# Slot 0 read without the plan, half of the plan and the zero blocks in the first layer, spare products on TensorE, and the first turns of the last stage in three banks

## The chip, the cores and the metric

The kernel runs on one core of a Trainium2 chip. The metric is the device time of one execution in microseconds (us). Besides the timed runs there is one profiled execution, whose trace gives all rows below. The engines are PE (TensorE, matrix products), DVE (VectorE), ACT (ScalarE), POOL (GpSimd) and SP (SyncE, which here only issues DMAs).

## The reference

A linear attention with decays, then two mixtures of experts. B, H, S, D = 4, 8, 768, 48, so N = 3072 tokens of 384 numbers; E = 8 experts, hidden width F = 1024.

```python
for t in range(S):                                  # attention
    cur = einsum('bhd,bhe->bhde', u[None] * kt, vt)
    y[:, :, t] = einsum('bhd,bhde->bhe', rt, state + cur)
    state = wt[:, :, :, None] * state + einsum('bhd,bhe->bhde', kt, vt)
...
expert_idx = argmax(logits, axis=1)                 # first layer: best expert of each token
for e in range(E):
    h = maximum(x[expert_idx == e] @ w1[e], 0.0)
    out[expert_idx == e] = gate_w[..., None] * (h @ w2[e])
...
order = argsort(-(x @ w_gate).flatten())            # second layer: pairs by falling logit,
for idx in order:                                   # each expert takes at most N // E tokens
    tok, e = idx // E, idx % E
    if assigned[tok] >= 0 or counts[e] >= cap: continue
    assigned[tok] = e; counts[e] += 1
for e in range(E):
    h = maximum(x[assigned == e] @ w1[e], 0.0)
    out[assigned == e] = h @ w2[e]
```

## The kernel before, in words

The program has three blocks, one behind the other. At the end of a block each engine drains and all five meet; only then does the next block begin. Each engine's program is written out by hand, in order, and engines wait for each other by semaphores. Nothing is planned by a scheduler.

**Attention (lines 153 to 815).** It runs over 24 tiles t of 128 tokens. SP loads decays, k and r, and v. DVE makes two scans of the decays (`scan_after`, `scan_before`), the scaled k (`decay_k`) and the masked scores. POOL makes the scaled r (`decay_r`, line 375). PE makes the scores (`score`, line 687), the outputs (`values`), the state and all turns. POOL begins with a list of constants (lines 330 to 367); only behind the last of them, at line 389, does its loop with `decay_r` begin. Every three tiles DVE chooses the best expert of each token (`choose`) and gives it its place among its expert's rows (`place`). POOL then scatters the rows by an indirect DMA into `sorted_rows` (line 384), which has a region of 3200 rows for each expert. `judge` (line 528) and the product at line 814 find out whether the decays are too wide for this method; if they are, `judged` (line 265) lets all engines run a general form instead. With these inputs it does not.

Behind the last tile DVE runs `plan_slots` (lines 101 to 142): 22 small chained instructions. A slot is a block of 128 rows of one expert, and there are up to 31. The plan gives each slot's expert and first row, each expert's last slot, and in `pad_row` the row behind each expert's last. `pad_regions` (line 145) waits for `pad_row` and stores a block of 128 zero rows behind each expert's rows: SP issues those of experts 0 to 3, ACT those of 4 to 7. SP waits until all eight have landed (line 319), POOL until the last scatters have landed (line 396).

**First layer (lines 1042 to 1337).** It runs over the slots i. SP first raises 26 semaphores (`signals`, line 1110). ACT loads the rows of slot i (`load_x`), whose first row it reads from `slot_row`. PE turns them (line 1275), DVE copies the turn out (line 1230), PE makes the 24 products of the hidden layer (line 1312, in two halves of 12, each product two records), ACT applies relu (line 1171), and PE makes the 8 products of the output (line 1328). DVE's program begins with two fills, `logits` and `tokens`.

**Second layer (lines 1348 to 1860).** It finds the assignment in 8 phases p, one expert each. In a phase DVE offers 31 thresholds at a time (`offer`), PE counts who reaches them (`count`, line 1722), DVE narrows (`narrow`), PE spreads the digit (`digit`, line 1728); four rounds make one threshold. Then PE ranks the members (`rank`), DVE builds `row_is` in two halves (line 1632), PE makes the token table from them (`tables`, line 1744), and POOL gathers the expert's rows from `y_rows` (line 1485). PE turns the three tiles i of 128 rows (`x_transposes`, line 1752), ACT copies them out (`x_evac`, line 1511), and PE makes the expert's two layers (`first`, line 1765, and `second`, line 1781), each product 384 wide. The search of phase p + 1 is written between the products of phase p. For phase 0 there is nothing to put it between. All turns go to the one bank `p_x`, so a turn waits until ACT has copied the last one out.

Of the kernel before, what the change touches and what calls it, by code (L numbers as in the profile page):

```python
# [80 lines left out]
def shared(nc, sb, ps, sem, io, keep):  # L81

    for name, shape, kind in (("ident", [P, P], F32), ("mask", [P, P], F32), ("tri", [P, P], BF16),
# [6 lines left out]
                              ("enT", [P, KD, E], F32), ("bad", [P, 1], I32), ("zeros", [P, ROW], F32),  # L90
# [10 lines left out]
def plan_slots(dve, keep, s_p):  # L101

    base, region, iota8, ones, steps, iota_s = (keep[n] for n in ("base", "region", "iota8", "ones", "steps", "iota_s"))
    slot_expert, slot_row, last_slot, pad_row = (keep[n] for n in ("slot_expert", "slot_row", "last_slot", "pad_row"))
    count, over, slots_of, end_of, start_of = (keep[n] for n in ("count", "over", "slots_of", "end_of", "start_of"))
    past, which, pick, tmp = (keep[n] for n in ("past", "which", "pick", "pick_tmp"))
    start_at, end_at, row_f = (keep[n] for n in ("start_at", "end_at", "row_f"))
    n = [0]

    def chain(ins):  # L110
        n[0] += 1
        ins.then_inc(s_p, 1)
        dve.wait_ge(s_p, n[0])

    by_slot = lambda a: a[:, :].unsqueeze(1).broadcast_to([P, SLOTS, E])
    by_expert = lambda a: a[:, :].unsqueeze(2).broadcast_to([P, SLOTS, E])
    chain(dve.tensor_tensor(count[:, :], base[:, :], region[:, :], ALU.subtract))
    chain(dve.tensor_copy(pad_row[:, :], base[:, :]))
# [4 lines left out]
    chain(dve.tensor_tensor(start_of[:, :], end_of[:, :], slots_of[:, :], ALU.subtract))  # L123
    chain(dve.tensor_tensor(past[:, :, :], by_expert(iota_s), by_slot(end_of), ALU.is_ge))
# [3 lines left out]
    chain(dve.tensor_tensor(pick[:, :, :], by_expert(which), by_slot(iota8), ALU.is_equal))  # L128
# [4 lines left out]

# [6 lines left out]

    chain(dve.tensor_copy(slot_row[:, SLOTS:SLOTS + 1], pad_row[:, E - 1:E]))
    chain(dve.tensor_copy(last_slot[:, :], end_of[:, :]))


def pad_regions(eng, experts, io, keep, s_p, s_pads):

    eng.wait_ge(s_p, 2)
# [5 lines left out]
def attention(nc, general, sb, ps, sem, io, keep):  # L153
# [3 lines left out]
    iota8, region, bad = (keep[n] for n in ("iota8", "region", "bad"))  # L157
# [27 lines left out]
    rows = sb("rows", [P, RB * G, ROW], F32)  # L185
# [8 lines left out]
    pos = sb("pos", [P, RB, G], U32)  # L194
# [15 lines left out]
    s_scale = sem("s_scale")  # L210
# [6 lines left out]
    s_votes = sem("s_votes")  # L217
    s_plan = sem("s_plan")
    s_pads = sem("s_pads")
    s_u = sem("s_u")  # L220
# [54 lines left out]
    with nc.Block() as block:  # L275
# [48 lines left out]
        def _(pool):  # L324
# [40 lines left out]
            for a in range(KD):  # L365
                const(pool.tensor_copy(keep["fold"][32 * a:32 * a + 32, :], ident[32 * a:32 * a + 32, 32 * a:32 * a + E]))
# [1900 lines left out]
```

## Time and profile before

| | us |
|---|---|
| median of 3 timed runs | 880.9 (879.58, 880.90, 883.29) |
| the profiled execution | 879.44 |
| its span, from the first to the last instruction | 877.7 |
| PE busy in the span | 805.9 (92%) |
| DVE busy | 432.7 (49%) |
| ACT busy | 319.2 (36%) |
| POOL busy | 122.4 (14%) |

The span starts at the first instruction; all times in rows count from there. The attention block lasts until about 195 us, the first layer until about 527, the second to the end. Busy times of PE are modelled from pipelined instructions, so a busy PE need not be at its peak.

### The profile page before, as it was taken

Reading aid. Unit: us, or ns where it says so; the run is one execution under the profiler, and the core shown is the slowest. Engines: PE = TensorE matmul, PEld = TensorE weight load, DVE = VectorE, ACT = ScalarE, POOL = GpSimd, SP = SyncE. Lnnn points to the kernel's source line nnn. Section 1 sums busy time; section 2 is a strip of 40 time slices with the busy share of each in tenths; the row PEclk is TensorE's granted clock in tenths of the full one; section 3 lists DMA queues with packets and bytes.
Section 4 is the critical chain, followed back from the end, with each engine's and each line's share of the span. In section 5 each row is a group of like instructions: output and inputs, shape, how many; then the busy total and the mean of one; then the engine's idle time right before and its main releaser. Section 6 shows DMA issues by size and latency. Waiting matters only on the chain. (4 is left out here: it accounts for less than half of the span.)

```text
span 877.7 us, 17862 instructions
## 1 busy us (share of the span) xinstructions
PE 805.9 (92%) x6212; PEld 584.4 (67%) x6213; DVE 432.7 (49%) x1259; ACT 319.2 (36%) x808; POOL 122.4 (14%) x146
## 2 busy tenths in 40 slices
PE   5999999929999999999999982399999999999996
PEld 4888888717877788877788862255565555655653
DVE  7799999742333333333333337664726364452000
ACT  3887788713344443344443340011111112122120
POOL 4123433320000000000000000102021010202201
PEclk9999999968999999999999995599999999999998
DMA  9446555735666555566564520513415051436100
GB/s 303 148 150 203 186 176 183 262 137 178 200 220 236 181 178 189 207 215 238 181 215 150 175 99 2 170 67 124 153 56 177 23 180 53 155 133 215 40 19 29
DMA packets 61918, 136.20 MB, mean 155 GB/s; under 512 B 4696, under 2 KB 36320, under 8 KB 61856
## 3 DMA queue, kind: packets, MB, share of 16 engines
q1 hardware_dynamic: 45536, 98.46, 32.6%
q0 software_dynamic: 6912, 23.75, 7.9%
q10 hardware_dynamic: 9408, 13.18, 4.7%
q8 instruction: 37, 0.61, 0.3%
q14 instruction: 25, 0.20, 0.1%
HBM read 117.48 MB, written 17.89 MB: 154 GB/s over the span
## 5 line engine op out<-in xcount | busy, mean ns | idle before, releaser
L1312 PEld LDWEIGHTS p_h<-x_t,w1s 128*128 128x128 f32 x1296 | 152.3, 193 | 8.0 <-issue 1.1
L1328 PE MATMUL p_o<-w2s,hid_t 128*128 x432 | 156.8, 497 | 0.0
L1312 PE MATMUL p_h<-x_t,w1s 128*128 128x128 f32 x1296 | 154.7, 276 | 0.8 <-DVE x_t L1230 0.8
L1765 PE MATMUL p_gh<-g_t,w1s 128*128 128x384 f32 x384 | 138.1, 506 | 0.7 <-ACT g_t L1511 0.7
L1781 PE MATMUL p_go<-w2s,g_hid 128*128 128x384 f32 x384 | 135.6, 496 | 0.0
L1328 PEld LDWEIGHTS p_o<-w2s,hid_t 128*128 128x128 f32 x432 | 75.8, 190 | 41.2 <-issue 5.2
L1171 ACT ACTIVATE hid_t<-p_h 128x512 f32<-128x512 f32 x54 | 32.2, 597 | 189.2 <-PE p_h L1312 189.2
L1765 PEld LDWEIGHTS p_gh<-g_t,w1s 128*128 128x128 f32 x384 | 71.1, 194 | 43.8 <-issue 5.3
L1781 PEld LDWEIGHTS p_go<-w2s,g_hid 128*128 128x128 f32 x384 | 70.5, 192 | 41.1 <-issue 1.4
L1525 ACT ACTIVATE g_hid<-p_gh 128x384 f32<-128x384 f32 x64 | 31.4, 490 | 122.8 <-PE p_gh L1765 122.8
L1485 POOL DMA_INDIRECT g_in<-y_rows,table x24 | 24.0, 1002 | 254.6 <-DVE table L1640 249.7
L687 PE MATMUL p_g<-r_dec,k_dec 64*128 64x128 f32 x384 | 43.8, 297 | 10.2 <-POOL r_dec L375 9.4
L1518 ACT ACTIVATE o_row<-p_go 128x384 f32<-128x384 f32 x24 | 11.8, 490 | 104.1 <-PE p_go L1781 104.1
L687 PEld LDWEIGHTS p_g<-r_dec,k_dec 64*128 64x128 f32 x384 | 39.0, 199 | 14.1 <-issue 12.6
L425 ACT ACTIVATE diag_v<-v_pad,diag 128x48 f32<-128x48 f32 x192 | 48.0, 327 | 0.0
L1578 DVE TENSOR_TENSOR filled<-p_search,room 31x8 f32<-31x8 f32 x28 | 4.3, 154 | 81.9 <-PE p_search L1722 74.8
L1137 POOL DMA_DIRECT2D w2s<-in_w x12 | 9.1, 757 | 250.2 <-PE p_o L1328 215.9
L375 POOL TENSOR_TENSOR r_dec<-kr_t,decays 128x512 f32<-128x512 f32 x24 | 28.5, 1187 | 104.4 <-issue 60.1
L1722 PEld LDWEIGHTS p_search<-takers,reach 128*31 128x31 bf16 x868 | 23.9, 96 | 25.3 <-DVE reach L1571 13.1
L1495 POOL DMA_INDIRECT out<-o_row,table x24 | 23.5, 978 | 121.6 <-ACT o_row L1518 121.3
L1238 DVE COPY lt<-p_route 96x128 f32<-96x128 f32 x27 | 7.8, 288 | 65.3 <-PE p_route L1290 65.3
L1230 DVE COPY x_t<-p_turn 128x384 f32<-128x384 f32 x28 | 15.6, 558 | 49.1 <-PE p_turn L1275 49.1
(258 smaller groups left out, 1108.3 us busy)
## 6 DMA issues: line engine op xcount, KB each, us to landing
w1s<-in_w SPq DMA_DIRECT2D x28, 1536.0 KB, 6.3
kr_t<-in_kr_t SPq DMA_DIRECT2D x24, 512.0 KB, 4.1
w1s<-in_w1b SPq DMA_DIRECT2D x8, 1536.0 KB, 6.4
w2s<-in_w2b SPq DMA_DIRECT2D x8, 1536.0 KB, 10.6
w2s<-in_w POOLq DMA_DIRECT2D x12, 768.0 KB, 6.7
w_pad<-in_w_t SPq DMA_DIRECT2D x24, 256.0 KB
v_pad<-in_v_pad SPq DMA_DIRECT2D x24, 256.0 KB, 4.3
x_in<-sorted_rows ACTq DMA_DIRECT2D x28, 198.0 KB, 2.5
```

Of the source, the lines that this page charges most:

```text
L375: pool.tensor_tensor(r_dec[:, t % 3, :, :], kr_t[:, q, 1, :, :], before[:, t % 2, :, 0:P], ALU.mult).then_inc(s_rdec, 1)
L425: ins = act.activation(diag_v[:, t % 2, h, :], v_pad[:, q, h, 0:D], ACT.Copy, scale=diag[:, t % 2, h:h + 1])
L687: ins = pe.matmul(p_g[g][:, a, :], k_dec[half, t % 2, a, :], r_dec[half, t % 3, a, :], start=True, stop=True)
L1171: act.activation(hid_t[:, half * g:half * (g + 1), :], p_h[g][:, :, :], ACT.Relu).then_inc(s_relu, 1)
L1312: ins = pe.matmul(p_h[g][:, m, :], w1s[:, q, a, f:f + P], x_t[:, q, a, :], start=(a == 0), stop=(a == KD - 1))
L1328: ins = pe.matmul(p_o[:, :], hid_t[:, m, :], w2s[:, bass.ds(half, 1), m, :].rearrange("p o n -> p (o n)"), start=(m == 0), stop=(m == KF - 1))
L1485: pool.indirect_dma_start(out=x_in[:, i, :], out_offset=None, in_=io["y_rows"][:, :], in_offset=place(0, p, i)).then_inc(s_in[i], 16)
L1495: pool.indirect_dma_start(out=io["out"][:, :], out_offset=place(1, p, i), in_=o_row[:, p % 2, i, :], in_offset=None).then_inc(s_out[p % 2] ...
L1525: act.activation(hid[:, m, :], p_h[(KF * p + m) % 3][:, :], ACT.Relu).then_inc(s_relu, 1)
L1722: ins = pe.matmul(p_c[0:CAND, :], reach[:, i, :], takers[:, i, :], start=(i == 0), stop=(i == SLOTS - 1))
L1765: ins = pe.matmul(p_h[n % 3][:, :], w1s[:, p % 2, a, m * P:(m + 1) * P], x_t[:, a, :], start=(a == 0), stop=(a == KD - 1))
L1781: ins = pe.matmul(p_o[n % 2][:, :], hid[:, m, i * P:(i + 1) * P], w2s[:, p % 2, m, :], start=(m == 0), stop=(m == KF - 1))
```

## The change

- POOL makes `tri`, `cand_0` and `fold` behind its first `decay_r` instead of before it (`later_constants`), and fills `logits` and `tokens` there, which DVE no longer does in the first layer.
- `keep_busy` issues spare f32 products of 128x128x128 whose results nobody reads: 20 at the start of attention, 20 behind the vote, 14 at the start of the first layer, 10, 5 and 15 around the first tables of the second layer.
- The plan is made in three parts: `plan_ends` (pad_row, one step), `plan_slots` (9 steps) in attention, and `plan_rows` (12 steps) at the start of the first layer. `judge` comes one turn later.
- In attention only the zero block of expert 0 is issued. The others are issued in the first layer: experts 1 to 3 by SP, before its first weights, 4 to 7 by ACT, behind the load of slot 0. Nobody waits in attention for the zero blocks or the last scatters to land; ACT waits for the scatters and the first zero block at the start of the first layer (`rows_stored`), and for the other seven before its loop.
- Slot 0 is loaded from row 0, without `slot_row`.
- The first layer's semaphores are made at the start and raised by SP within attention.
- In the second layer the three turns of phase 0 go to three banks (`p_x` and the two of `p_o`) and do not wait for ACT's copies; the first comes before `digit(1, 0)`.

```diff
+def rows_stored(eng, s_sc, s_first_pad):
+    for k, signal in enumerate(s_sc):
+        eng.wait_ge(signal, 16 * len(range(k, NT, RB * G)))
+    eng.wait_ge(s_first_pad, 16)
+def keep_busy(pe, n, into, one):
+    for _ in range(n):
+        pe.matmul(into, one[:, :], one[:, :], start=True, stop=True)
+def chained(dve, s_p, made):
+    n = [made]
     def chain(ins):
         n[0] += 1
         ins.then_inc(s_p, 1)
         dve.wait_ge(s_p, n[0])
+    return chain
+def plan_ends(dve, keep, s_p):
+    chained(dve, s_p, 0)(dve.tensor_copy(keep["pad_row"][:, :], keep["base"][:, :]))
 def plan_slots(dve, keep, s_p):
+    chain = chained(dve, s_p, 1)
     chain(dve.tensor_tensor(count[:, :], base[:, :], region[:, :], ALU.subtract))
-    chain(dve.tensor_copy(pad_row[:, :], base[:, :]))
...
+    chain(dve.tensor_copy(last_slot[:, :], end_of[:, :]))
+ROW_STEPS = 12
+def plan_rows(dve, keep, s_p):
...
-def pad_regions(eng, experts, io, keep, s_p, s_pads):
-    eng.wait_ge(s_p, 2)
+def pad_regions(eng, experts, io, keep, s_pads):
# attention, sync
-            pad_regions(sp, range(E // 2), io, keep, s_plan, s_pads)
-            sp.wait_ge(s_pads, 16 * E)
             sp.wait_ge(s_clear, 16)
+            for signal in credited:
+                sp.sem_inc(signal, CREDIT)
+            sp.wait_ge(s_plan, 1)
+            pad_regions(sp, range(1), io, keep, s_first_pad)
             judged(sp, "sync")
# attention, gpsimd: later_constants, called behind decay_r(0)
-            pool.wait_ge(s_shape, 2)
...
+            def later_constants():
+                pool.wait_ge(s_shape, 2)
+                pool.tensor_copy(tri[:, :], mask[:, :]).then_inc(s_shape, 1)
+                const(pool.tensor_scalar(keep["cand_0"][:, :], keep["cand_n"][:, :], 1.0 / 16, 1.0, ALU.mult, ALU.subtract))
+                pool.wait_ge(s_const, 26)
+                for a in range(KD):
+                    const(pool.tensor_copy(keep["fold"][32 * a:32 * a + 32, :], ident[32 * a:32 * a + 32, 32 * a:32 * a + E]))
+                pool.wait_ge(s_const, 29)
+                const(pool.memset(keep["logits"][:, :, :], NEG))
+                const(pool.memset(keep["tokens"][:, :], 0.0))
+                pool.wait_ge(s_const, 31)
...
                 if t + 2 < NT:
                     decay_r(t + 2)
+                if t == -2:
+                    later_constants()
                 if t >= G + 3:
                     scatter(t - G - 3)
-            for t in range(NT):
-                if t + RB * G >= NT:
-                    pool.wait_ge(s_sc[slot(t)], 16 * (t // (RB * G) + 1))
             judged(pool, "gpsimd")
# attention, scalar
-            act.wait_ge(s_in, 32)
+            act.wait_ge(s_in, 48)
...
-            pad_regions(act, range(E // 2, E), io, keep, s_plan, s_pads)
             judged(act, "scalar")
# attention, vector
-                if t == NT:
+                if t == NT + 1:
                     judge()
-            dve.wait_ge(s_votes, 1)
+            plan_ends(dve, keep, s_plan)
+            dve.wait_ge(s_narrow, 3)
             dve.tensor_scalar(bad[:, :], p_d[:, 0, 0:1], float(P), None, ALU.is_lt).then_inc(s_narrow, 1)
             plan_slots(dve, keep, s_plan)
# attention, tensor
-            pe.wait_ge(s_u, 16)
-            pe.wait_ge(s_shape, 3)
+            pe.wait_ge(s_const, 1)
+            keep_busy(pe, 20, p_y[:, 0, :], ones)
+            pe.wait_ge(s_in, 48)
+            pe.wait_ge(s_shape, 2)
...
-            pe.matmul(p_d[:, 0, 0:1], ones[:, :], narrow[:, NT:NT + 1], start=True, stop=True).then_inc(s_votes, 1)
+            pe.matmul(p_d[:, 0, 0:1], ones[:, :], narrow[:, NT:NT + 1], start=True, stop=True).then_inc(s_narrow, 1)
+            keep_busy(pe, 20, p_y[:, 0, :], ones)
# first layer, sync
-            for signal in signals:
-                sp.sem_inc(signal, CREDIT)
+            pad_regions(sp, range(1, E // 2), io, keep, s_pads)
# first layer, scalar
-            load_x(0, 0, 0, True)
+            rows_stored(act, keep["s_sc"], keep["s_first_pad"])
+            act.dma_start(x_in[:, 0, :], io["sorted_rows"][0:P, :]).then_inc(s_xin[0], 16)
+            pad_regions(act, range(E // 2, E), io, keep, s_pads)
             norm(0, 0, 0)
+            act.wait_ge(s_plan, ROW_STEPS)
+            act.wait_ge(s_pads, 16 * (E - 1))
             last = loop(act, body)
# first layer, vector
-            dve.memset(logits[:, :, :], NEG).then_inc(s_init, 1)
-            dve.memset(tokens[:, :], 0.0).then_inc(s_init, 1)
-            dve.wait_ge(s_init, 2 + CREDIT)
+            plan_rows(dve, keep, s_plan)
             x_evac(0, 0)
# first layer, tensor
+            keep_busy(pe, 14, p_h[1][:, 0, :], ident)
             pe.wait_ge(s_wg, 16)
             x_transposes(0, 0, 0)
# second layer
+    turned_in = lambda p, i: (p_x if p > 0 or i == 0 else p_o[i - 1])[:, :]
...
-            def tables(p):
+            def tables(p, spare=0):
                 for i in range(SLOTS):
                     if i in (HALVES[0][0], HALVES[1][0]):
+                        if i > 0:
+                            keep_busy(pe, spare, p_h[2][:, 0:P], ident)
                         pe.wait_ge(s_facts, 2 * p + (1 if i == 0 else 2))
...
             def x_transposes(p, i):
                 pe.wait_ge(s_in[i], 16 * (p + 1))
-                if TE * p + i > 0:
+                if p > 0:
                     pe.wait_ge(s_xev, TE * p + i)
...
-            tables(0)
+            keep_busy(pe, 10, p_h[2][:, 0:P], ident)
+            tables(0, 5)
+            keep_busy(pe, 15, p_h[2][:, 0:P], ident)
             count(1, 0)
+            x_transposes(0, 0)
             digit(1, 0)
-            for i in range(TE):
+            for i in range(1, TE):
                 x_transposes(0, i)
```

## Rows read from the trace of the kernel before

**Rows 1.** The page, the span in 40 equal slices, busy tenths:

```profile
PE   5999999929999999999999982399999999999996
```

**Rows 2.** Stretches: us, busy us (instructions) of PE, PEld, DVE, ACT, POOL; granted clock; DMA:

```profile
182.00:183.00 1.00, 0.18 (x6) 0.18 (x7) 0.66 (x4) 0.00 (x0) 0.54 (x1) 0.63 0.36 128
202.00:203.00 1.00, 1.00 (x7) 1.00 (x7) 0.00 (x0) 0.00 (x0) 0.00 (x0) 0.63 1.03 418
526.00:528.00 2.00, 0.36 (x2) 0.30 (x2) 0.98 (x3) 0.00 (x0) 0.00 (x0) 0.75 0.00 0
574.00:576.00 2.00, 2.00 (x16) 1.02 (x15) 0.36 (x1) 0.17 (x1) 0.00 (x0) 0.80 0.00 0
```

**Rows 3.** Timeline of the start: start, duration, engine, line, operation, count, [idle before <- released by]:

```profile
4.22 1.13 POOL L361 CAST tri<-mask 128x128 bf16<-128x128 f32 x1
5.88 2.10 POOL L366 COPY fold<-ident 32x8 f32<-32x8 f32 x3
8.07 1.19 POOL L375 TENSOR_TENSOR r_dec<-kr_t,decays 128x512 f32<-128x512 f32 x1
8.30 2.05 DVE L541 TENSOR_TENSOR_SCAN decays<-w_pad,last 128x520 f32<-128x520 f32 x1 [0.36 <-DMA w_pad<-in_w_t]
9.40 3.06 PE L687 MATMUL p_g<-r_dec,k_dec 64*128 64x128 f32 x16 [9.40 <-POOL r_dec L375]
14.70 3.09 PE L687 MATMUL p_g<-r_dec,k_dec 64*128 64x128 f32 x16
23.35 1.71 PE L687 MATMUL p_g<-r_dec,k_dec 64*128 64x128 f32 x16
```

**Rows 4.** POOL's drain at the three block ends: duration min/median/max ns, start us:

```profile
L275 POOLq DRAIN  x1: 2032/2032/2032, 192.8 to 192.8; - x1
...
L1107 POOLq DRAIN  x1: 1035/1035/1035, 453.7 to 453.7; - x1
...
L1456 POOLq DRAIN  x1: 3974/3974/3974, 873.5 to 873.5; - x1
```

**Rows 5.** Timeline, POOL's last DMA in each of the three blocks:

```profile
187.08 0.96 POOL L384 DMA_INDIRECT sorted_rows<-rows,pos  x1 [0.30 <-issue]
...
446.62 0.75 POOL L1137 DMA_DIRECT2D w2s<-in_w  x1 [5.92 <-DMA w2s<-in_w]
...
870.13 0.96 POOL L1495 DMA_INDIRECT out<-o_row,table  x1 [4.20 <-ACT o_row L1518]
```

**Rows 6.** Timeline from attention to the first layer:

```profile
185.56 4.56 ACTq L150 DMA_DIRECT2D sorted_rows<-zeros  x4
...
195.76 0.36 ACTq L1152 DMA_DIRECT2D x_in<-sorted_rows  x1
...
198.28 0.87 PE L1275 MATMUL p_turn<-ident,x_in 128*128 128x128 f32 x3 [14.63 <-DMA x_in<-sorted_rows]
...
199.92 6.94 PE L1312 MATMUL p_h<-x_t,w1s 128*128 128x128 f32 x48 [0.77 <-DVE x_t L1230]
...
215.20 2.84 PE L1312 MATMUL p_h<-x_t,w1s 128*128 128x128 f32 x24
```

**Rows 7.** Timeline of phase 0 and the first products of the second layer:

```profile
551.79 4.36 DVE L1632 TENSOR_TENSOR row_is<-row_b,iota_p 128x2048 bf16<-128x2048 bf16 x2
...
556.21 0.57 PE L1744 MATMUL p_rows<-facts_at,row_is 128*128 128x12 bf16 x15 [1.47 <-DVE row_is L1632]
...
560.76 0.90 PEld L1722 LDWEIGHTS p_search<-takers,reach 128*31 128x31 bf16 x31 [4.08 <-DVE reach L1571]
...
563.80 0.37 SPq L1471 DMA_DIRECT2D w2s<-in_w2b  x1
...
567.00 2.90 PE L1765 MATMUL p_gh<-g_t,w1s 128*128 128x384 f32 x4 [0.67 <-ACT g_t L1511]
...
575.73 0.93 PE L1722 MATMUL p_search<-takers,reach 128*31 128x8 bf16 x31
...
586.59 4.12 PE L1765 MATMUL p_gh<-g_t,w1s 128*128 128x384 f32 x12
```

More of the change, by code:

```diff
@@ L98, in shared @@
         keep[name] = sb(name, shape, kind)
[L101 to L108, printed above, removed]
+def rows_stored(eng, s_sc, s_first_pad):
[7 more added lines that the diff above has]
+    n = [made]
     def chain(ins):
@@ L113, in chain, with plan_slots @@
         dve.wait_ge(s_p, n[0])
-    by_slot = lambda a: a[:, :].unsqueeze(1).broadcast_to([P, SLOTS, E])
-    by_expert = lambda a: a[:, :].unsqueeze(2).broadcast_to([P, SLOTS, E])
+    return chain
+def plan_ends(dve, keep, s_p):
+    chained(dve, s_p, 0)(dve.tensor_copy(keep["pad_row"][:, :], keep["base"][:, :]))
+def plan_slots(dve, keep, s_p):
+    base, region, ones, steps, iota_s = (keep[n] for n in ("base", "region", "ones", "steps", "iota_s"))
+    slot_expert, last_slot, count, over = (keep[n] for n in ("slot_expert", "last_slot", "count", "over"))
+    slots_of, end_of, past, which = (keep[n] for n in ("slots_of", "end_of", "past", "which"))
+    chain = chained(dve, s_p, 1)
     chain(dve.tensor_tensor(count[:, :], base[:, :], region[:, :], ALU.subtract))
-    chain(dve.tensor_copy(pad_row[:, :], base[:, :]))
     chain(dve.tensor_tensor(over[:, :, :], count[:, :].unsqueeze(2).broadcast_to([P, E, NT]),
@@ L253, in attention @@
     s_place = sem("s_place")
-    s_sc = [sem(f"s_sc{i}", False) for i in range(RB * G)]
+    s_sc = keep["s_sc"]
     CHOOSE, PLACE = 5, 5
@@ L1039, in route_any, with first_signals @@
     return {"sync": on_sync, "gpsimd": on_gpsimd, "scalar": on_scalar, "vector": on_vector, "tensor": on_tensor}
+FIRST = ("init", "expert", "turn", "xt", "xtev", "h", "relu", "o", "y", "yt", "ytev", "lt", "ltev", "lg",
+         "lgdone", "gate", "ssq", "root", "arg", "exp")
+FIRST_PAIRS = ("xin", "xfree", "out")
+FIRST_PLAIN = ("w2", "plan")
+def first_signals(sem):
+    sem.made()
+    made = {n: sem(f"f_{n}") for n in FIRST}
+    made.update({n: [sem(f"f_{n}{i}") for i in range(2)] for n in FIRST_PAIRS})
+    made.update({n: sem(f"f_{n}", False) for n in FIRST_PLAIN})
+    made["credited"] = sem.made()
+    return made
 def first_layer(nc, sb, ps, sem, io, keep):
@@ L1143, in _, with load_x @@
         def _(act):
-            def load_x(i, q, turn, first=False):
+            def load_x(i, q, turn):
                 row = act.value_load(slot_row[0:1, bass.ds(i, 1)], min_val=0, max_val=E * REGION - P)
-                if not first:
-                    act.wait_ge(s_xt, i - 1 + CREDIT)
+                act.wait_ge(s_xt, i - 1 + CREDIT)
                 act.wait_ge(s_xfree[q], turn + CREDIT)
@@ L2198, in program @@
                 "s_w": [sem(f"s_w{i}", False) for i in range(2)],
+                "s_sc": [sem(f"s_sc{i}", False) for i in range(RB * G)], "s_first_pad": sem("s_first_pad", False),
+                "s_pads": sem("s_pads", False), "first": first_signals(sem),
                 "s_slot": [sem(f"s_slot{i}", False) for i in range(2)], "s_wg": sem("s_wg", False)}
```

97 lines of the change are left out of this document (38 added, 59 removed).

## The prediction

> **What bounds the kernel now.** I read the page's 40 slices first, then the busy-time view by stretches, the timeline of the three places where TensorE (PE) stands still, and last the queue records at the ends of the blocks. In the slices [rows 1] PE is full except in three places: the first slice, slices 8 to 9 (attention gives way to the first layer) and slices 24 to 25 (the first layer gives way to the second). Everywhere else the kernel is bound by PE, so only these three places can pay. At each, two things cost time: PE waits, and then it works at the lower of its two levels. The stretches show that: the granted clock goes from 1.00 to 0.50 at 182.4 us and comes back at 202.7, goes again at 527 and comes back at 574.8 [rows 2]. Half of 2.4 GHz is 1.2 GHz, and the rows agree: 12 products of 128x128x128 in f32 (24 records) take 2.84 us at the high level, 0.24 us each; the first 384-wide ones take 1.3 us each (2.90 us for 4 records, their last end overlapping) against 0.69 us (4.12 for 12) [rows 6, 7]. So a 128-wide spare product costs about 0.24 us at the high level and, doubled, 0.47 us at the low one (estimate). The level rose 2.8 us after dense work began at 199.92, and 7.8 us after it began at 567.00; I take these as ends for every rise. The profile's clock column says 1.00 in the first 22 us too, but the rows deny it: one tile's 16 score records take 3.06 and 3.09 us there and 1.71 us at 23.35 [rows 3]. I go by the rows.
>
> **Place 1, the start.** Edits: most constants of POOL go behind the first r_dec, 20 spare products run on PE before the first score, the small waits change. POOL's first r_dec starts at 8.07, right behind the constants that ended at 7.98; what it needs from VectorE (DVE) is ready at about 6.8, where DVE's second scan ends and its k_dec begins. So it ends near 8.0 instead of 9.26, and the first scores start at 8.1 instead of 9.40: 1.3 us. The 20 spare products start when `ones` is filled (1.07) and end at 1.1 + 2.8/2 + 4.7 = 7.2 if the level rises early, at 9.7 if it rises 7.8 us on, at 10.6 if never. So the scores start between 8.1 and 9.7, and at the high level (1.7 us instead of 3.06). What is late next is POOL: the moved group (tri, cand_0, fold: 4.22 to 7.98, 3.8 us) plus two fills of logits and tokens (about 0.4 us by POOL's other fills) now stand between r_dec 0 and r_dec 1, which comes at 8.0 + 4.2 = 12.2 and ends at 13.4. The second scores start there instead of at 14.70: again 1.3 us. The third scores start at 23.35 now; with PE at the high level the chain through DVE (scans, normalize, masks, k_dec) would let them start near 20.2, with PE at the low level only near 22. The gain of the place is thus 1.3 to 3.2 us; below, 0 if the spare products outlast the first r_dec at the low level. Between these PE has holes of 1 to 2 us, so I do not count on the high level throughout: 2.6 us. ScalarE's wait for 48 instead of 32 holds back only its squares and the y_rows clearing, for one small load; nothing there is on the path.
>
> The second scan row is 2.05 us at 8.30, beside r_dec (8.07 to 9.26), where other scans take 1.24 [rows 3]. The Trainium skill, page "GPSIMD Engine Reference", section Specifications, says that POOL shares its SBUF interfaces with VectorE and contends with DVE instructions that read two SBUF inputs. By that rule r_dec 0, moved to 6.8, would now stretch k_dec or rk by up to 1.2 us instead of the scan; place 1 would come to 2.0 to 2.6 us by it. The trace agrees in this one row.
>
> **Place 2, attention to first layer.** Now: DVE makes the whole plan until 190.9, ACT and SP issue four zero blocks each (4.56 us), SP waits until they have landed, POOL waits until the scatters have landed, then all engines meet; x_in is issued at 195.76, turned at 198.28, and the first products start at 199.92 and run at the low level until 202.7 [rows 6]. After: DVE issues `pad_row` first, then 10 plan steps; its last is at about 187, and no engine waits for a landing inside the block. The obvious sum is a meeting near 189 to 191, 4 to 5 us earlier. I do not take it, because of the drains. POOL's drain is the last to end before the meeting: 192.8 + 2.03 = 194.8 [rows 4]. At the three block ends the drain lasts 2.03, 1.04 and 3.97 us, but it ends 7.7, 8.1 and 7.4 us after the start of POOL's last DMA (187.08, 446.62, 870.13) [rows 4, 5]. A drain that only had a length would not line up like that; one that waits for something of the last software DMA would. The last scatter moves only as far as `choose` does, 0.2 us for the `judge` put one turn later. So the meeting comes at 186.9 + 7.4 = 194.3 (bounds 190.3, if the drain is just 1.0 us behind a branch done at 189.0; and 195.0). Engines that now stop waiting at 187 to 191 only wait there instead.
>
> From 194.4: ACT passes its ten landing waits (all landed by 191), issues x_in at about 194.7, landed 2.45 us later at 197.1. But PE has 14 spare products in front of the turns. The 20 behind the votes run from 183.2 to 188.9 to 192.7, end before the meeting, and leave PE still for 2 to 5 us, so I expect the low level again at 194.4. Fourteen then take 3.3 us plus half of the time to the rise: 2.8 gives 199.1, 5 gives 200.2, never gives 201.0. I take 199.6. The turns follow in 0.5 us, DVE's evacuation in 0.6 (its 12 row steps, at most 5 us, ended at 199.4 or before), the first products at 200.9, at the high level. Now the first tile's 48 records end at 206.86; after, 200.9 + 24 x 0.24 = 206.7. Gain 0.1 us, bounds -1.2 and 6. The spare products only turn slow useful time into slow useless time.
>
> The new waits: ACT has four zero blocks (4.7 us) and the wait for seven landings before its loop, so relu 0 and x_in 1 stand behind it: issued until 199.7, landed 2.5 to 3.1 us later, x_in 1 issued at about 203.8, relu at 204.5. PE needs relu only at 206.7 and x_in 1 at 210.6, so there is cover of 2 us; if the meeting is early but PE is fast, cover stays, since both move. DVE's wait for the vote stands before the plan, but the vote's product ends near 183.6, before `pad_row` is made. SP has three zero blocks before its w1 load, but 26 semaphore increments less; w1 for tile 1 is needed after 211. The Trainium skill, page "DMA: Bandwidth & Descriptors", section "Issuing engines are not separate DMA queues", says that all queues interleave on the same engines. By that rule the seven zero blocks, now issued around x_in 0 instead of before it, can delay it; the spare products end 2.5 us after it should land and would hide that, so the sum stays.
>
> **Place 3, first layer to second.** Ten spare products start behind the rank at 549.1 (5.0 us before the tables' first product) and need 2.4 to 4.7 us; DVE gives the first half of row_is at 554.0, halfway through its two (551.79 + 4.36) [rows 7]. Dense for up to 4.7 us, they should raise the level near 552 to 554. The five between the halves take 1.2 us (2.4 low) after 554.7; the second half is ready at 556.15, so they cost nothing high, 1 us low. Fifteen follow the tables at 556.8 and end at 560.4 (high) or 563.9 (low); the next count waits for DVE's reach until 560.76 [rows 7]. Then the three turns, each into its own bank, no longer wait for ScalarE's copy (0.49 us) in between. They wait only for the gathers: the last landed at 563.8, when SP was released for w2. So last turn at 564.3, copy 564.9, first products at 565.0 instead of 567.00: 2.0 us. At the high level the six wide products, one count and one digit that now fill 567.00 to 575.73 take 6 x 0.69 + 1.4 = 5.5 us, not 8.7: 3.2 more. DVE's search keeps pace there (2.0 us from digit to reach, against 2.1 us of three products). Sum 5.2 us; bounds -2 (all low) and 5.7. From there PE is full to the end, so it stays.
>
> **Sum.** 2.6 + 0.1 + 5.2 = 7.9 us. The profiled execution took 879.44 us (span 877.7 and 1.7 around it), so 871.5; the median of the timed runs, 880.9, is 1.5 above it, so I forecast 873.0.
>
> **Rivals.** (a) The drain is not tied to the last DMA. The meeting comes at about 191, PE's spare products nearly join and the level holds, first products at about 195.5: place 2 gives 5.5 instead of 0.1, time 867.6. For it: one drain is only 1.04 us. Against: three ends within 0.8 us of one another. (b) The level lapses again between spare and real work: in the holes at 10 to 13 us, and between 560.4 and 565.0, where PE has one count and three turns. The falls at 182.4 and 527 came while PE still did scattered work, before it stood still altogether, which speaks for it. Place 1 gives 1.3, place 2 -0.8, place 3 2.7: 3.2 us, 877.7. (c) Slower: the spare products never raise the level soon enough and stand before ready work. 20 end at 10.6 (-1.3), 14 let the turns begin at 201.0 (-2.6), 5 and 15 push the count from 560.7 to 564.9 and the products to 569 (-2): 886.8. It decides if the rise comes later than about 6 us after dense work begins at all three. Against it: the rise at 2.8 us. (d) The gathers land as before, later turns wait for them and the change does nothing at place 3 but the level: part of my own range.
>
> **Chances.** Forecast 0.45 (own range 870 to 876), (a) 0.22, (b) 0.26, (c) 0.07. Within 0.5% (876.5 to 885.3, about what a measurement can tell from no change) lies most of (b); so faster 0.72, same 0.21, slower 0.07. Range 866 to 879: it leaves out (c), the edge of (b), and the best of (a).
>
> **What would show it.** Right: score records of about 1.7 us at 8 to 10 us; POOL's drain ends over 7 us after its last scatter starts and ends last; x_in landed but PE in spare products behind the block; first 384-wide products about 5 us earlier, measured from the second layer's start, at clock 1.00. Wrong: a drain of about 1 us and a meeting at 191; a granted clock of 0.50 behind the spare products; turns that begin later than the data.

## The result, and the profile after

The changed kernel takes 874.7 us (median of 17 runs, 870.1 to 882.4) where the kernel before takes 881.8 (17 runs, 879.6 to 884.3): ratio 0.9925, 95% interval [0.9906, 0.9944], 7.1 us. The profiled execution took 874.32 us, span 872.6 against 877.7. The forecast was 7.9 us and 873.0. The sum was right; two of its three terms were not, and the third only in part. That the sum came out is luck.

The page's slices, PE and the granted clock, answer to [rows 1]:

```profile
PE   8999999979999999999999983899999999999996
PEclk8999999989999999999999995799999999999998
```

The two bad places inside the span are still in the same slices. Slice 8 (the ninth digit) went from 2 to 7 tenths busy, mostly with spare products, which are no work.

**Place 1.** Timeline of the start of the changed kernel (start us, duration, engine, line, operation, count, [idle before <- released by]); compare [rows 3]:

```profile
1.14 7.35 PE L111 MATMUL p_y<-ones 128*128 128x128 f32 x40 [1.14 <-POOL ones L360]
...
6.91 1.48 POOL L407 TENSOR_TENSOR r_dec<-kr_t,decays 128x512 f32<-128x512 f32 x1 [2.74 <-DVE decays L580]
7.25 1.69 DVE L597 TENSOR_TENSOR rk<-kr_t 128x512 f32<-128x512 f32 x1
8.54 1.68 PE L717 MATMUL p_g<-r_dec,k_dec 64*128 64x128 f32 x16
...
12.80 1.37 DVE L589 TENSOR_TENSOR k_dec<-kr_t,decays 128x512 f32<-128x512 f32 x1
14.09 0.68 DVE L597 TENSOR_TENSOR rk<-kr_t 128x512 f32<-128x512 f32 x1
14.22 3.09 PE L717 MATMUL p_g<-r_dec,k_dec 64*128 64x128 f32 x16 [2.48 <-DVE k_dec L589]
...
23.51 1.80 PE L717 MATMUL p_g<-r_dec,k_dec 64*128 64x128 f32 x16
```

The spare products raised the level (the clock of TensorE), and the first scores take 1.68 us instead of 3.06. Then PE stands still from 11.7 to 14.2, the level falls there (at 13.5), and the second scores take 3.09 as before. The third start at 23.51 against 23.35: nothing is left of the place.

**Place 2.** Queue records of POOL's drains at the ends of attention and of the kernel (compare [rows 4]); below them the handover's timeline, answering to [rows 5, 6]:

```profile
L301 POOLq DRAIN  x1: 4540/4540/4540, 186.9 to 186.9; - x1
...
L1488 POOLq DRAIN  x1: 3969/3969/3969, 868.4 to 868.4; - x1
```

```profile
187.47 0.96 POOL L416 DMA_INDIRECT sorted_rows<-rows,pos  x1 [0.30 <-issue]
...
191.69 3.36 PE L111 MATMUL p_h<-ident 128*128 128x128 f32 x28 [1.36 <-PEq L301]
192.02 0.37 ACTq L1209 DMA_DIRECT2D x_in<-sorted_rows  x1
193.13 4.23 ACTq L179 DMA_DIRECT2D sorted_rows<-zeros  x4
195.01 0.52 PE L1305 MATMUL p_turn<-ident,x_in 128*128 128x128 f32 x3
197.04 5.60 PE L1342 MATMUL p_h<-x_t,w1s 128*128 128x128 f32 x48 [1.51 <-DVE x_t L1262]
201.06 0.36 ACTq L1180 DMA_DIRECT2D x_in<-sorted_rows  x1
201.52 0.60 ACT L1199 ACTIVATE hid_t<-p_h 128x512 f32<-128x512 f32 x1 [3.21 <-issue]
208.02 2.84 PE L1342 MATMUL p_h<-x_t,w1s 128*128 128x128 f32 x24
```

The drain ends at 191.4, 3.9 us after the last scatter starts, and not 7.4 or more. The level held from the 20 spare products to the 14, and the first tile takes 5.60 us instead of 6.94. The second tile starts at 208.02 instead of 212.19, and the second layer 3.9 us earlier (523.62 for 527.56).

**Place 3.** Timeline of the second layer's start in the changed kernel, answering to [rows 7], and below it stretches of it (columns as in [rows 2]; the third from the end is the granted clock):

```profile
544.65 4.61 PE L111 MATMUL p_gh<-ident 128*128 128x128 f32 x20
...
552.30 3.59 PE L111 MATMUL p_gh<-ident 128*128 128x128 f32 x30
556.46 0.93 PE L1754 MATMUL p_search<-takers,reach 128*31 128x8 bf16 x31 [0.56 <-issue]
...
559.34 0.68 PE L1786 MATMUL p_go<-ident,g_in 128*128 128x128 f32 x3 [0.61 <-DMA g_in<-y_rows,table]
...
560.69 2.90 PE L1799 MATMUL p_gh<-g_t,w1s 128*128 128x384 f32 x4 [0.67 <-ACT g_t L1543]
```

```profile
550.00:558.00 8.00, 7.01 (x105) 6.37 (x102) 6.34 (x14) 0.10 (x1) 3.31 (x3) 1.00 0.38 125
560.00:562.00 2.00, 1.33 (x3) 0.84 (x3) 0.11 (x1) 0.49 (x1) 0.00 (x0) 0.50 0.74 143
569.00:571.00 2.00, 2.00 (x35) 1.08 (x33) 0.00 (x0) 0.49 (x1) 0.00 (x0) 0.78 0.00 0
```

The turns no longer wait for a copy, only the third for its gather. The first wide products start 37.07 us after the layer instead of 39.44. But the level, high from 549.4, fell just before them, and they take 2.90 us as before. The 2.4 us gained there do not all stay: from the second layer's start to the end of the span are 348.96 us instead of 350.14, 1.2 less.

### The profile page after: what moved, and what is told of

Same layout as the page of the kernel before. It is cut to its first block and busy times, and to the rows that moved or that the text cites. A ratio compares the mean times of both kernels' runs of the same rounds, so it can differ in the third digit from the quotient of the medians.

```text
span 872.6 us, 18191 instructions
## 1 busy us (share of the span) xinstructions
PE 829.4 (95%) x6380; PEld 607.4 (70%) x6381; DVE 432.9 (50%) x1257; ACT 319.4 (37%) x808; POOL 123.0 (14%) x148
```

## The experiments

All are compared with the kernel before on the same chip. Three chips served, one for each group of four, and the kernel before takes 878.9, 878.0 and 882.7 us on them: compare ratios, not times, from one group to the next.

### What the spare products, the start, the search and POOL's waits are worth

e1, the spare products set to none:

```
     for _ in range(0):          # was range(n)
         pe.matmul(into, one[:, :], one[:, :], start=True, stop=True)
```

> The changed kernel with all 84 spare products left out, everything else as in the change. Theory (the handover gains by the waits that went, the level is a second, smaller part): POOL's drain still ends near 191.4 us and x_in still lands near 195, so the first products of the first layer start near 196.2, but at the low level, and the ramp costs 1.4 to 3 us; the second layer's first products start near 2.0 us earlier than before, measured from its first instruction, at the low level. Sum 4 to 5 us under the kernel before, about 877. Rival (the spare products carry the change): without them no more than 1 us is left of the 7, about 881. If the drain theory of the forecast held, the meeting would be at 194.3; the trace after already has 191.4, and this run should show the same.

Measured: 872.4 us, ratio 0.9923 [0.9898, 0.9949], against 0.9925 for the change. All 84 spare products together are worth nothing that shows; the intervals leave room for some 2 us either way. Of the two expectations neither has the time: more is left than the 4 to 5 us of the theory. The drain ends at 190.8.

e2, the start as it was (the two fills stay behind the first r_dec):

```
-            pe.wait_ge(s_const, 1)
-            keep_busy(pe, 20, p_y[:, 0, :], ones)
...
     tri, cand_0 and fold made ahead of decay_r(0) again
```

> The changed kernel with the start of attention put back: tri, cand_0 and fold before the first r_dec, no 20 spare products before the first scores; the fills of logits and tokens stay behind r_dec 0. Theory (the start gives nothing, since r_dec beside VectorE's two-input instructions stretches these, 1.69 instead of 0.68 us for rk and 1.37 for k_dec, and the level lapses at 13.7 us): the same time as the changed kernel within 1 us, about 874.7, and tile 20 of attention at the same point, 174.2 us. Rival (the start gives the 1.3 to 3 us of the forecast in most runs, and the profiled run was an unlucky one): 1.5 to 3 us slower than the changed kernel, about 877.

Measured: 871.4 us, 0.9915 [0.9889, 0.9941]: the start's edits bring nothing that shows in the time.

e3, the search as it was (no fills, all turns through p_x, after the digit, each waiting for the last copy):

```
-            keep_busy(pe, 10, p_h[2][:, 0:P], ident)
-            tables(0, 5)
-            keep_busy(pe, 15, p_h[2][:, 0:P], ident)
+            tables(0)
...
-    turned_in = lambda p, i: (p_x if p > 0 or i == 0 else p_o[i - 1])[:, :]
+    turned_in = lambda p, i: p_x[:, :]
...
```

> The changed kernel with the second layer put back: no spare products (10, 5, 15), all three turns through one bank, after the digit. Theory: place 3 is worth 1.7 us when the level lapses before the first wide products, as in the profiled run after, and up to 5.2 when it holds; over many runs 2 to 3.5 us, so this kernel is at about 877.5. It should also vary less from run to run, about as the kernel before (5 us from lowest to highest) and not as the changed one (12 us), if the spread comes from the level at place 3. Rival: the place gives 5.2 us in nearly all timed runs and the profiled one was an exception: about 880.

Measured: 873.8 us, 0.9933 [0.9908, 0.9957]. By the ratios the place brings 0.7 us, and the intervals leave room for nothing as for 3 us; the rival, nearly all of the 5.2 us, is out.

e4, POOL waits for the scatters inside attention again:

```
+            for t in range(NT):
+                if t + RB * G >= NT:
+                    pool.wait_ge(s_sc[slot(t)], 16 * (t // (RB * G) + 1))
             judged(pool, "gpsimd")
```

> The changed kernel with one wait put back: POOL waits in attention until the last scatters have landed, as before, and then judges and drains. Theory A (the drain runs beside the landing when nobody waits for it; waiting first puts the landing, the load of `bad` and the drain one behind the other): the drain starts near 192 and ends near 194, the meeting moves from 191.5 to about 194, and the 14 spare products find the low level; 2.5 to 4.5 us slower than the changed kernel, about 878. Theory B (the drain ends a fixed time after the last scatter's landing or issue, whoever waits): the drain gets shorter by as much as it starts later and ends near 191.5; same time as the changed kernel.

Measured: 872.9 us, 0.9910 [0.9875, 0.9945]. The drain of e4 has the length that it had before:

```profile
L301 POOLq DRAIN  x1: 2037/2037/2037, 191.0 to 191.0; - x1
```

x_in 0 is issued 6.7 us after the last scatter's start instead of 4.5, but no time is lost that can be measured. Something behind the meeting takes back what the meeting gives.

### What takes it back, and what the drain costs

e5, the seven other blocks of zeros asked for at attention's end (SP three, ACT four) and waited for where they were:

```
             pad_regions(sp, range(1), io, keep, s_first_pad)
+            pad_regions(sp, range(1, E // 2), io, keep, keep["s_pads"])
...
+            act.wait_ge(s_plan, 1)
+            pad_regions(act, range(E // 2, E), io, keep, keep["s_pads"])
             judged(act, "scalar")
...
```

> The changed kernel, with the seven other blocks of zeros asked for at the end of attention (SP experts 1 to 3, ACT 4 to 7), and still waited for only ahead of ACT's loop. Theory (half of the handover's gain is given back on ACT: four issues and the wait for seven landings stand ahead of the load of tile 1's rows and of the first relu): ACT is at its loop before the first wide products end, the row load of tile 1 starts near 198.5 instead of 201 to 203, PE no longer stands still between the first and second wide products of tile 0 (1.0 to 2.0 us in runs so far), the second tile starts 1 to 2 us earlier against the first wide product, and the time is 0.1 to 0.3% shorter than the changed kernel's. Rival (ACT's wait is hidden behind the products as the prediction had it): first-to-second tile distance unchanged, same time. Second rival (the early blocks delay POOL's scatters, whose end the drain waits for): the meeting moves later than 191.5 and the gain goes.

Measured: 871.1 us, 0.9917 [0.9904, 0.9930]. Theory and second rival are both right, and cancel. Its rows, drain first:

```profile
L302 POOLq DRAIN  x1: 6512/6512/6512, 185.4 to 185.4; - x1
```

```profile
184.14 4.59 ACTq L179 DMA_DIRECT2D sorted_rows<-zeros  x4
...
186.04 0.96 POOL L418 DMA_INDIRECT sorted_rows<-rows,pos  x1 [0.31 <-issue]
...
192.57 0.36 ACTq L1211 DMA_DIRECT2D x_in<-sorted_rows  x1
...
201.26 0.60 ACT L1201 ACTIVATE hid_t<-p_h 128x512 f32<-128x512 f32 x1 [5.20 <-PE p_h L1343]
```

ACT is ready when PE is: relu waits for p_h again, no longer PE for relu. From the issue of x_in 0 to the second tile's first products are 16.5 to 16.7 us in the three kernels with early zeros (e5, e8, e11), and 18.4 on average, 16.0 to 20.3, in the nine with late ones. But beside the blocks the scatters take longer to land, and the drain waits for them: x_in 0 goes out 6.5 us after the last scatter's start.

e6, an explicit drain ahead of the last three scatters, and one ahead of the kernel's last transfer:

```
                 if t >= G + 3:
+                    if t - G - 3 == NT - G:
+                        pool.drain()
                     scatter(t - G - 3)
...
                 for i in range(TE):
+                    if TE * p + i == TE * E - 1:
+                        pool.drain()
                     pool.wait_ge(s_oev, TE * p + i + 1)
```

> The changed kernel with an explicit drain on POOL ahead of the last four scatters of attention, where POOL waits anyway, and one ahead of the last transfer of the second layer. Theory (POOL's drain costs some 83 ns for each software DMA since the last drain: 12 took 1.04 us, 24 took 2.04, 48 took 3.97): the new drains last about 1.7 us and 3.9 us where POOL stands still, the drain at the end of attention ends about 1 us after the last scatter has landed (meeting near 189.5 instead of 191.5), the last drain of the kernel shrinks from 3.97 to about 0.1 us, and the time is 4 to 6 us (0.5 to 0.7%) shorter than the changed kernel's. Rival (the length is tied to the block or to a fixed time after the last DMA): the drain at a block's end stays at 4.5 and 3.97 us, and the time stays.

Measured: 870.5 us, 0.9908 [0.9890, 0.9926]. (Three scatters stand behind the new drain in attention, not the four of the expectation.) The kernel's last drain shrank from 3.97 to 0.14 us. The one at attention's end did not, with 3 transfers instead of 24 since the last drain:

```profile
L301 POOLq DRAIN  x1: 4859/4859/4859, 186.9 to 186.9; - x1
```

It ends 0.18 us after the last scatter has landed. In the eight kernels that drain 24 transfers with the last still in flight and have its landing in the trace (changed, e1, e2, e3, e5, e9, e11, e12) it ends 1.03 to 1.04 us after it. So the count does matter there, with about half of its full 2.03 us: that much of the theory is right. But nothing is gained. The explicit drain holds back the last three scatters (POOL is idle for 3.43 us before them, 2.25 in the changed kernel), and the last one takes 4.2 us to land instead of 2.6 to 2.9 in seven kernels with late zeros and no such drain. Why it takes longer is open.

e7, the handover's part of the change alone: start (but for the two fills) and search as before, no spare products.

> Of the change only the handover to the first layer is left: POOL doesn't wait for scatters at the end of attention, only the first block of zeros is made there, half of the plan is made in the first layer; the constants stand where they stood, no spare products anywhere, and the last stage starts as before. Theory (all that the change brings is at the handover): ratio to the kernel before 0.992 to 0.995, like the whole change. Rival (the total is a sum of small gains of all three places): ratio 0.996 or more.

Measured: 874.2 us (12 runs, 872.8 to 880.6), 0.9962 [0.9947, 0.9977]: about half of the change. The rival fits better, though the interval reaches into the theory's range; yet e2 and e3, each without one of the two other places, lose nothing that shows. Its profiled execution is its slowest and is used for distances within a place alone.

e8, e5 and e6 together, without the start's edits and the spare products.

> The changed kernel without spare products and with the constants where they stood at the start, with the zeros asked for early and the two explicit drains. Theory (the gains of the two edits add up): 866 to 869 us where the kernel before takes 879 to 881, ratio near 0.985. Rival (they don't add): the ratio of the better of the two.

Measured: 870.4 us, 0.9920 [0.9908, 0.9933]. The rival is right, the interval leaves out the theory's 0.985. The explicit drain in attention lasts 5.87 us from 181.3 and holds back the last three scatters: POOL is idle for 4.28 us before them.

### The level at the start, and the drain alone

e9, the changed kernel again.

> The changed kernel once more, as it is, to stand beside the three others on one chip. Both theories expect the ratio 0.991 to 0.994 to the kernel before. In the profile: PE stands still between 11.7 and 14.2 us, the level falls there and the scores of tile 1 take 3.09 us.

Measured: 877.2 us (9 runs, 870.5 to 880.3), 0.9919 [0.9891, 0.9946]. Here the second and third scores both ran at the low level (3.09 and 3.10 us), and the handover shows the new wait at its worst:

```profile
200.37 5.60 PE L1342 MATMUL p_h<-x_t,w1s 128*128 128x128 f32 x48 [1.88 <-issue]
208.11 5.83 PE L1358 MATMUL p_o<-w2s,hid_t 128*128 x12 [2.15 <-ACT hid_t L1199]
213.77 0.49 PE L1305 MATMUL p_turn<-ident,x_in 128*128 128x128 f32 x3
```

```profile
206.74 0.36 ACTq L1180 DMA_DIRECT2D x_in<-sorted_rows  x1
207.20 1.08 ACT L1199 ACTIVATE hid_t<-p_h 128x512 f32<-128x512 f32 x2 [5.46 <-issue]
...
213.33 0.53 ACT L1188 ACTIVATE f_square<-x_in 128x384 f32<-128x384 f32 x1 [3.33 <-DMA x_in<-sorted_rows]
```

ACT reaches relu at 207.20, PE has waited 2.15 us for it, the level falls (granted clock 0.63 from 208 to 212), and x_in 1, asked for at 206.74, lands only at 213.3.

e10, the kernel before with the one explicit drain at its end (the second half of e6's diff).

> The kernel before with one explicit drain on POOL ahead of the last transfer of the second layer, nothing else. Theory (a drain costs some 83 ns for each software DMA since the last one, here 47 of 48, and it is on the path only at the kernel's end): the last drain takes 0.14 us instead of 3.97, the end moves 3.5 us nearer to the last output row, and the time is 3 to 4 us shorter: ratio 0.9955 to 0.9965. Rival (what the drain no longer waits for is waited for elsewhere at the end, or the explicit drain delays the last transfer by more than it saves): ratio 0.999 or more.

Measured: 879.1 us against 882.7, 0.9951 [0.9931, 0.9970]. The new drain and the last:

```profile
L1491 POOLq DRAIN  x1: 5087/5087/5087, 867.4 to 867.4; - x1
```

```profile
L1456 POOLq DRAIN  x1: 142/142/142, 877.0 to 877.0; - x1
```

From the start of ACT's last output row (872.03; 869.36 in the kernel before) to the end of the span are 5.4 us instead of 8.3. That is 3.0 us nearer and not 3.5: the rival is right in part, since the new drain ends at 872.49 and the last transfer starts 1.6 us after the row's start, not 0.8. The time follows: this gain is real, the interval leaves out 1, and it is apart from the change.

e11, the changed kernel with e5's edit, this drain and ten more spare products ahead of the second scores (e12's diff).

> The changed kernel with the zeros asked for early, the explicit drain ahead of the kernel's last transfer only (none in attention), and ten more spare products between the first tile's turns of k and the second tile's scores. Theory (the gains add up): 3.5 us from the end, 1 to 1.5 from the zeros, 1 to 2 from the start, so 6 to 7 us under the changed kernel, ratio to the kernel before 0.984 to 0.987. Rival (only the end's gain survives): ratio 0.988 to 0.989.

Measured: 872.8 us, 0.9875 [0.9843, 0.9907], the lowest ratio of all, 4.3 us under e9 on the same chip, though the intervals overlap. It lies between the theory and the rival; the interval takes in both.

e12, the ten more spare products alone:

```
                 if t + 1 < NT and (t + 1) % C < C - 1:
                     k_transposes(t + 1)
+                if t == -1:
+                    keep_busy(pe, 10, p_y[:, 0, :], ones)
```

> The changed kernel with ten more spare products on PE ahead of the second tile's scores, where PE stands still from 11.7 to 14.2 us. Theory (place 1 gave nothing because the high level lapsed in that stretch, and not because DVE or the loads bound the start): the scores of tile 1 take 1.7 us instead of 3.09, those of tile 2 start 1 to 2 us earlier than 23.5, and every later tile with them; the time is 1 to 2 us shorter. Rival (DVE and the loads bound the first tiles): scores of tile 1 are short, but those of tile 2 start at 23.3 to 23.6 as before, and the time stays.

Measured: 874.5 us, 0.9898 [0.9879, 0.9917], 2.7 us under e9, whose interval overlaps. The timeline of its start shows the theory right:

```profile
11.78 2.40 PE L111 MATMUL p_y<-ones 128*128 128x128 f32 x20
14.44 1.71 PE L717 MATMUL p_g<-r_dec,k_dec 64*128 64x128 f32 x16 [0.26 <-DVE k_dec L589]
...
21.31 1.71 PE L717 MATMUL p_g<-r_dec,k_dec 64*128 64x128 f32 x16 [1.08 <-DVE k_dec L589]
```

The hole is filled, the level holds, and the third scores start at 21.31, 2.2 us before the changed kernel's, with DVE as the bound now. In e11 the level falls again at 22.8, and the fourth scores start at 29.69; in e12 it holds, and they start at 28.24 (changed: 30.53).

### The places over all profiles

One profile is one execution, so the places are read over all fourteen. Columns: start of the third scores (us); from the last scatter's start to the issue of x_in 0, and to the second tile's first products; from the second layer's start to its first wide products, and to its first output row.

```
kernel          scores  x_in 0  tile 1   wide   row 0
before           23.35    8.68   25.11  39.44   69.2
e10 before+drain 24.79    8.72   25.44  39.44   69.3
changed          23.51    4.55   20.55  37.07   67.5
e9 changed again 23.69    4.39   24.66  36.93   64.8
e1 no spare      23.72    4.28   22.73  37.20   65.1
e2 undo start    23.54    4.54   21.95  36.97   64.8
e3 undo search   23.63    4.57   24.56  39.05   68.7
e4 POOL waits    23.60    6.69   25.00  37.33   67.2
e5 early zeros   22.48    6.53   23.19  37.65   68.2
e6 drain twice   22.70    5.02   23.47  37.32   67.2
e7 handover only 24.87    4.53   22.82  39.03   68.9
e8 both edits    25.02    5.24   21.79  37.33   65.2
e11 all          21.32    7.04   23.66  38.19   68.1
e12 bridge       21.31    4.47   22.73  38.29   68.4
```

Start: 24.3 on average over the five kernels with the old start (before, e10, e2, e7, e8), 23.3 over the six with spare products as in the change (changed, e3, e4, e5, e6, e9): 1.0 us. The five alone spread over 1.7 us, so this is a guess at the size and no more. Nor do the third scores tell all: in e7 and e9 they too run at the low level, and the fourth start at 35.31 and 34.12. Handover: x_in 0 is 4.2 us earlier in the eight kernels with the change's waits (changed, e1, e2, e3, e6, e7, e9, e12: 4.5 on average), but the second tile 2.3 us (22.9 on average, 20.6 to 24.7, against 25.3). Search: the wide products come 1.8 us earlier (37.4 over ten, against 39.2 over the four with the old search), whether or not there are spare products. That makes 5.1 us. The pair of profiles has 5.1 too, but by chance, from other parts: 3.9 up to the second layer's start and 1.2 behind it. The timed medians say 7.1, and the 2 us between lie within the interval (4.9 to 8.3 us).

## Why the prediction came out right, and where it was wrong

**What bounds the kernel.** Right: only the three places moved. From the second tile's products to the second layer's start is 315.4 to 315.8 us in all fourteen profiles.

**Place 1: 2.6 us forecast, 0 in the profile, 1.0 on average.** The step that failed is "I do not count on the high level throughout: 2.6 us". It set the price of the holes too low, and their size: "holes of 1 to 2 us" was the premise. The hole of 2.5 us ahead of the second scores took the level away, and with it the later gain; e12 shows that filling it gives 2.2 us more. The forecast of 20.2 for the third scores at the high level compares with 21.31. r_dec 0 did move (from 8.07 to 6.91), but lasted 1.48 us and stretched rk from 0.68 to 1.69; r_dec 1 did the same to k_dec (1.37). Each of the two ends 0.55 us after the r_dec that it stood beside. The Trainium skill, page "GPSIMD Engine Reference", section Specifications, says that POOL contends with DVE instructions that read two SBUF inputs: the trace agrees, and the 1.0 us on rk is within the "up to 1.2" worked out for it.

**Place 2: 0.1 us forecast, 4.2 in the profile, 2.3 on average.** Two steps failed, in opposite directions. The first is "one that waits for something of the last software DMA would" line up. That three drains end 7.4 to 8.1 us after a DMA's start was a coincidence of three blocks with different waits in them. The lengths alone tell more: 12, 24 and 48 software transfers cost 1.04, 2.03 and 3.97 us, 83 to 87 ns each. e6 and e10 show it at the kernel's end (one transfer left: 0.14 us), e4 fits it (24 transfers, all landed: 2.04). With transfers in flight the drain ends a little after the last landing, 1.04 us with 24 of them (changed: 191.4). So something of the last DMA does count, but its landing, 2.9 us after its start here, and not an end 7.4 us on. So rival (a) was right on the meeting. With the meeting so early the 20 and the 14 spare products nearly joined, and the level held between them in the changed kernel and in e2, e3, e9 and e12. In e4, e5, e6 and e11, where x_in 0 goes out 0.5 to 2.6 us later, it fell for 3.4 us and was back before the first products.

The second is "there is cover of 2 us; if the meeting is early but PE is fast, cover stays". It did not. PE waits 0.3 to 2.2 us for relu in seven of the nine kernels that wait for late zeros (not in the changed kernel's own profile, nor in e1's), and x_in 1 then takes up to 6.7 us to land beside the loads of w1. The working had "landed 2.5 to 3.1 us later" for it; yet in the kernel before it took 6.25 us (issued at 200.16), where it was asked for early enough. The Trainium skill, page "DMA: Bandwidth & Descriptors", section "Issuing engines are not separate DMA queues", was weighed for x_in 0 alone; what it says of shared engines bore on x_in 1 and, in e5, on the scatters.

**Place 3: 5.2 us forecast, 2.4 in the profile at the first products, 1.8 on average.** The first step, 2.0 us from the turns and gathers, was right at the first products. The second, 3.2 us from the high level, failed. The eight kernels with fills at the search all show the level up before the wide products and down again 35 to 37 us after the layer's start, just ahead of them. In six it came back at 45 to 47, in two (e2, e9) at 40. With the new turns and no fills (e1, e8) it rose once, at 40 to 41, during those products, and with the old search, which has no fills either, at 47; here are e8's first wide products and the two stretches around the rise:

```profile
565.09 2.90 PE L1803 MATMUL p_gh<-g_t,w1s 128*128 128x384 f32 x4 [0.67 <-ACT g_t L1547]
```

```profile
556.00:566.00 10.00, 5.15 (x58) 3.62 (x59) 6.25 (x17) 1.47 (x3) 3.31 (x3) 0.50 0.30 79
567.00:569.00 2.00, 2.00 (x34) 1.06 (x33) 0.09 (x1) 0.00 (x0) 0.00 (x0) 0.72 1.06 399
```

The first output row comes after 69.0 us on average with the old search, after 65.1 and 65.2 with the new turns alone, and after 67.0 on average with fills as well (64.8 to 68.4). So in the profiles the turns are worth some 3.9 us there, and the fills rather cost some 2 of them. Two profiles stand against eight, and the medians do not prove it. That the gain of this place stays to the end, as the forecast had it, holds in part only (1.2 of 2.4 us in the pair).

**The sum** was right because errors cancelled: 1.6 and 3.4 us too much at places 1 and 3, 2.2 too little at place 2 (averages). What is left, 2.8, is the step from 7.9 to the 5.1 of the profiles; the timed medians, at 7.1, were kinder. The changed kernel's profile has rival (a) at the meeting and rival (b)'s lapses at both other places. Neither was given a joint chance, though they do not exclude each other.

**Left open.** In the profiles of before, changed, e9, e10, e11 and e12 the second layer's second output row comes 9.4 to 9.6 us after the first, in the other eight after 6.5; e9 to e12 all ran on one chip, e1 to e8 on two others; the chip of the first pair is not known. It does not go with the edit. In those six, DVE goes on only 1.7 us after the count that it needs, for a cause outside of the engines' rows, and the level then falls for 3.4 us; here is the changed kernel, below it e1:

```profile
596.29 0.15 DVE L1610 TENSOR_TENSOR filled<-p_search,room 31x8 f32<-31x8 f32 x1 [4.24 <-remote]
```

```profile
593.76 0.15 DVE L1610 TENSOR_TENSOR filled<-p_search,room 31x8 f32<-31x8 f32 x1 [2.53 <-PE p_search L1754]
```

What holds DVE there is open. Why the level comes back sooner or later was not tried apart from the fills.

## What to carry to other kernels

Spare products bought nothing here as long as a hole was left between them and the real work, and 2.2 us, in the profile, at the one place where it was filled: price the whole stretch up to the real work, not the fill. Before moving a wait, list what stands on the same engine behind it; here four issues and seven landings moved ahead of ACT's first relu and gave back nearly half of the gain. Where one cost has several readings, ask of each what it says of the length as well as of the end, and look for a cheap edit that splits them: the drain went by a count and by a landing, and one explicit drain, nearly all of it where POOL stood idle, gave 3.5 us.

## What the runs showed of the hardware

- POOL's drain takes 83 to 87 ns for each of its software transfers since the last drain, even long after they have landed (12: 1.04 us, 24: 2.03, 48: 3.97, in the kernel before). With transfers in flight it ends after the last landing: by 1.04 us with 24 of them (eight profiles), by 0.9 with 21 and by 0.2 with 3 (e6, e8).
- An explicit drain ahead of the kernel's last transfer takes 5.09 us and leaves 0.14 us at the end (e10); it holds back that transfer by 0.8 us.
- The contention goes both ways: beside DVE's k_dec and rk, r_dec took 1.48 us instead of 1.19 (changed kernel).
- Seven 198 KB blocks of zeros beside the last scatters moved the drain's end by about 2 us (e5).
- A load of 198 KB took 6.25 us beside the loads of w1 in the kernel before, where the load ahead of it took 2.4 (x_in 1 and x_in 0).
- The changed kernel spreads over 12 us in 17 runs, the kernel before over 5, and the slower runs have the lower mean clock in the main (correlation -0.79). e12, with the same fills at the search, spreads over 1.7 us in six, so where the spread comes from is not shown.
